# Masks, exponentials and reciprocals of an attention pair, spread over three successive steps of an attention and MoE kernel

## Chip, cores and metric

One core of a Trainium2 chip. The time is the device time of one execution, in microseconds; a lower time is better. The profile is one execution, with its own time.

## What is computed

```python
# windowed attention: 4 batches, 8 heads, 576 positions, head_dim 64
scores = scale * q @ k.T                       # only 0 <= row - col < 64 is kept
attn = exp(scores - max) / (sum(exp) + 1e-9)
x = (attn @ v) as rows                         # 2304 x 512
# gated product without a nonlinearity
x = ((x @ w1) * (x @ w2)) @ w3 @ w_out         # 512 -> 1024 -> 1024 -> 512
# top-1 of 8 experts
e = argmax(x @ w_gate); s = softmax prob of e * sigmoid(x @ w_output_gate)[e]
out = s * (relu(x @ ew1[e]) @ ew2[e])          # 512 -> 1024 -> 512
```

## The kernel before

Every large product is made of three matmuls (`product3`): each float32 operand is split in a high part (h, made by ScalarE as a rounding copy) and a low part (l, what is left, made by the vector engine or, for four pieces of w2 and two of w1, by GpSimd). A tile that ScalarE, the vector engine and TensorE hand round therefore passes ScalarE (copy), vector engine (subtract), and then TensorE.

Attention works in **pairs**: two heads by two blocks side by side, 3 windows of 64 rows each, six pairs p = 0 to 5 to a batch. A pair passes these calls:

- `score(p)`, TensorE: 24 small matmuls into two banks
- `masks(p)`, vector engine, L1002: for each of two halves a scaled sum with the mask (sm, L1011) and a lay (prob, L1015), then the negated row maxima (nmx, L1017). `score(p + 1)` waits until both sm of p have left the banks.
- `exps(p)`, ScalarE, L814: six exponentials with their sums (L818)
- `weigh(p)`, vector engine, L1032: 1e-9 added to the sums (L1035), reciprocals (rec, L1037)
- `normal(p)`, GpSimd, L1440: prob times rec (L1443)
- `turn(p)`, TensorE, L581: three transposes of prob; `turn_out(p)`, vector engine, four products into pT (L1027)
- `value(p)`, TensorE, L590: 24 small matmuls; `value_hi(p)` (ScalarE, L823) and `value_lo(p)` (vector engine, L1041) split the result into x, transposed. `value(p + 1)` waits for `value_lo(p)`.

The attention of the first batch lies in the **fold stage** (29 to 98 us and a little ahead of it). There TensorE multiplies w3 with w_out in 16 half products (`w_order`, steps i), each of which ScalarE and the vector engine split into Wh and Wl; meanwhile w3, w1 and w2 are loaded and split too (`hi_w3`, `lo_w3`, `hi_w12`, `lo_w12`). The other three batches lie each in a **chunk** of 384 rows of x (there are six chunks; three carry no attention). A chunk has 14 steps e: eight hidden tiles (e = 0 to 7), then six row tiles. In hidden tile f TensorE makes the two products of x with w1 and w2; ScalarE copies the first (a_sb, L890), the vector engine multiplies the second with it (ab_f, L1140), ScalarE rounds (abh, L892), the vector engine subtracts (abl, L1142). A row tile (L655) runs over eight parts f of abh and abl with W; in the first one TensorE waits, part by part, for abl of tile f. Row tiles of the kind n = 1 come first (e = 8 to 10); their result is copied out by the vector engine, that of n = 0 by ScalarE.

Every engine runs its own list of calls, in order, and waits on semaphores. The order is written by hand, by functions from the step to the pair whose call stands behind (or ahead of) the step's own work:

| call | engine | pair in step e, before |
|---|---|---|
| score | TensorE | 0 ahead of step 0; e/2 + 1 at even e |
| masks | vector engine | 0 ahead of step 0; e/2 + 1 at even e |
| exps | ScalarE | 0 ahead of step 0; e/2 + 1 at even e |
| weigh | vector engine, ahead of the step's own work | 0 at e = 1; e/2 at even e from 2 |
| turn, turn_out | TensorE, vector engine | e/2 - 1 at even e from 2 |
| value, value_hi, value_lo | TensorE, ScalarE, vector engine | e/2 - 2 at even e from 4; the last in step 13 |

In the fold stage the same holds for e = i - 2, with a few steps written out (`fold_scored`, `fold_weighed`). GpSimd's `normal` follows `fold_weighed` there, and `lo_w12` stands behind it in the steps 3, 6, 8, 10, 11 and 12. In a chunk GpSimd has only the `normal` calls and the stores of x. SyncE issues the loads; they wait for scores and values that have left their buffers. Within a step the vector engine takes its own work, then turn_out, value_lo, masks; ScalarE its own work, value_hi, exps.

Of the kernel before, what the change touches and what calls it, by code (L numbers as in the profile page):

```python
# [29 lines left out]
def build(nc, B, H, S, qT_in, kT_in, v_in, w1, w2, w3T_in, w_out, w_outT, w_gates, ew1, ew2, out):  # L30
# [41 lines left out]
    with ctx:  # L72
# [192 lines left out]
        def scored(e):  # L265
            return e // 2 + 1 if e % 2 == 0 and e // 2 + 1 < NP else None
# [4 lines left out]
        def valued(e):  # L271
            return e // 2 - 2 if e % 2 == 0 and e >= 4 else None

        def weighed(e):
            return 0 if e == 1 else e // 2 if e >= 2 and e % 2 == 0 and e // 2 < NP else None

        LAST = NP - 1

# [29 lines left out]
        def row_bank(cc, i):  # L308
            return bank[(2 * cc + i) % 4]
# [7 lines left out]
        def fold_scored(i):  # L317
            return i - 2 if i in (2, 3) else scored(i - 2) if i > 3 else None

        def fold_weighed(i):  # L320
            return {3: 0, 5: 1}.get(i, i // 2 - 1 if i >= 6 and i % 2 == 0 and i // 2 - 1 < NP else None)


        w3_steps = {1: 3, 5: 4, 7: 5, 9: 6, 11: 7}
# [12 lines left out]
        def w_bank(i):  # L337
            return bank[i % 4]
# [470 lines left out]
        def _(act):  # L809
# [4 lines left out]
            def exps(b, p):  # L814
                act.wait_ge(nmx_ok, b * NP + p + 1)
                for i in range(6):
                    pr, c = prob[p % 2][:, i * WIN:(i + 1) * WIN], p % 2 * 6 + i
                    ex_i = act.activation(pr, pr, ACT.Exp, bias=nmx[:, c:c + 1], accum_out=sums[:, c:c + 1])  # L818
                ex_i.then_inc(exp_ok, 1)
# [34 lines left out]
            for i, (it, n) in enumerate(w_order):  # L854
                def own():
                    first, end = PARTS[n]
                    if i == 3:
                        act.wait_ge(g1_done, 1)
                        for j in range(0, KF, 2):
                            g = act.activation(woh_pair(j, DM, WXC), bank[4][:, j * LG:(j + 2) * LG].rearrange("p (j c) -> p j c", c=LG),  # L860
                                               ACT.Copy)
                        g.then_inc(g1_hi, 1)
                    act.wait_ge(W_done, w_count(it, n))
                    act.activation(Wh[:, it * WXC + first:it * WXC + end], w_bank(i)[:, 0:end - first],
                                   ACT.Copy).then_inc(W_hi, 1)

                if i == len(w_order) - 1:
                    value_hi(0, LAST, 0)
                own()
                if i >= 2 and valued(i - 2) is not None:  # L870
                    value_hi(0, valued(i - 2), 0)
                if i in w3_steps:
                    hi_w3(w3_steps[i])
                if i == 2:
                    hi_wo(1)
                if fold_scored(i) is not None:
                    exps(0, fold_scored(i))
                if i in w12_steps:
                    hi_w12(w12_steps.index(i))

# [6 lines left out]
            def chunk(cc, c, batches, b, parity, final):  # L887
                def hidden_tile(f):
                    act.wait_ge(a_done, cc * KF + (f + 1))
                    act.activation(a_sb[f % 2][:, :], hidden_bank(cc, f, 0)[:, 0:CH], ACT.Copy).then_inc(a_ok, 1)  # L890
                    act.wait_ge(ab_ok, cc * KF + (f + 1))
                    act.activation(abh[:, f * CH:(f + 1) * CH], ab_f[f % 2][:, :], ACT.Copy).then_inc(ab_hi, 1)  # L892

                def row_tile(i, n, tt):
                    if n == 0:
                        act.wait_ge(xA_done, cc * CT + (tt + 1))
                        act.wait_ge(x_free, cc + 1)
                        act.activation(x_sb[tt][:, 0:HALF], row_bank(cc, i)[:, 0:HALF], ACT.Copy).then_inc(xA_ok, 1)

                def attend(e):  # L900
                    if b is not None and valued(e) is not None:
                        value_hi(b, valued(e), parity)
                    if b is not None and scored(e) is not None:
                        exps(b, scored(e))

                if b is not None:
                    exps(b, 0)
                for f in range(KF):
                    hidden_tile(f)
                    attend(f)  # L910
                if final:
                    for part in range(2):
                        for p in range(NP1):
                            split_hi(0, part, p)
                            if (part, p) == (1, 1):
                                xs_out(0, bank[7])
                for n, tt, i in row_tiles:
                    if b is not None and KF + i == NSTEP - 1:
                        value_hi(b, LAST, parity)
                    row_tile(i, n, tt)  # L920
                    attend(KF + i)
# [76 lines left out]
        def _(dve):  # L998
# [79 lines left out]
            for i, (it, n) in enumerate(w_order):  # L1078
                if i == 3:
                    dve.wait_ge(const_ok, 2)  # L1080
                if i == 2:
                    dve.wait_ge(const_ok, 1)

                def own():
                    if i - 1 in w3_steps:
                        lo_w3(w3_steps[i - 1])
                    if i == 3:
                        lo_wo(1)
                    if fold_weighed(i) is not None:
                        weigh(0, fold_weighed(i))  # L1090
                    if i >= 1:
                        weight_splits(i - 1)
                    first, end = PARTS[n]
                    if i == 3:
                        dve.wait_ge(g1_hi, 1)
                        for j in range(0, KF, 2):
                            g = wo_lo_out(j, DM, WXC, bank[4][:, j * LG:(j + 2) * LG].rearrange("p (j c) -> p j c", c=LG))
                        g.then_inc(g1_lo, 1)
                    dve.wait_ge(W_hi, w_count(it, n))
                    ws = slice(it * WXC + first, it * WXC + end)  # L1100
                    dve.tensor_tensor(Wl[:, ws], w_bank(i)[:, 0:end - first], f32(Wh[:, ws]), ALU.subtract).then_inc(W_lo, 1)

                if i == len(w_order) - 1:
                    value_lo(0, LAST, 0)
                own()
                if i >= 2 and turned(i - 2) is not None:
                    turn_out(0, turned(i - 2), 0)
                    turn_out(0, turned(i - 2), 1)
                if i >= 2 and valued(i - 2) is not None:
                    value_lo(0, valued(i - 2), 0)  # L1110
                if fold_scored(i) is not None:
                    masks(0, fold_scored(i))
            weight_splits(len(w_order) - 1)


# [5 lines left out]
            def chunk(cc, c, batches, b, parity, final):  # L1121
# [4 lines left out]
                def attend(e):  # L1126
                    if b is not None and turned(e) is not None:
                        turn_out(b, turned(e), 0)
                        turn_out(b, turned(e), 1)
                    if b is not None and valued(e) is not None:  # L1130
                        value_lo(b, valued(e), parity)
                    if b is not None and scored(e) is not None:
                        masks(b, scored(e))

                def hidden_tile(f):
                    weights(f)
                    fc = slice(f * CH, (f + 1) * CH)
                    dve.wait_ge(b_done, cc * KF + (f + 1))
                    dve.wait_ge(a_ok, cc * KF + (f + 1))
                    dve.tensor_tensor(ab_f[f % 2][:, :], hidden_bank(cc, f, 1)[:, 0:CH], a_sb[f % 2][:, :], ALU.mult).then_inc(ab_ok, 1)  # L1140
                    dve.wait_ge(ab_hi, cc * KF + (f + 1))
                    dve.tensor_tensor(abl[:, fc], ab_f[f % 2][:, :], f32(abh[:, fc]), ALU.subtract).then_inc(ab_lo, 1)  # L1142

                def row_tile(i, n, tt):
                    weights(KF + i)
                    if n == 1:
                        dve.wait_ge(xB_done, cc * CT + (tt + 1))
                        dve.wait_ge(x_free, cc + 1)
                        dve.tensor_copy(x_sb[tt][:, HALF:DM], row_bank(cc, i)[:, 0:HALF])
                        dve.tensor_copy(L[:, bass.ds(cc * (CT * LG) + tt * LG, LG)], row_bank(cc, i)[:, HALF:HALF + LG]).then_inc(xB_ok, 1)  # L1150

                if b is not None:
                    masks(b, 0)
# [415 lines left out]
```

## Time and profile before

| | us |
|---|---|
| median of 3 runs (lowest, highest) | 752.13 (749.43, 752.37) |
| the profiled execution | 752.49 |
| its span, first to last instruction | 750.7 |
| TensorE busy | 711.7 |
| vector engine / ScalarE / GpSimd busy | 372.8 / 266.7 / 120.1 |

The mean granted TensorE clock of the span is 0.979 of full speed. The table shows how much each engine has to do, not who waits for whom; a time in the rows counts from the span's start. The fold stage ends near 98 us, the three chunks with attention run from 98 to about 171, from 222 to about 295 and from 295 to about 368, the last chunk ends near 475, and the expert stage takes the rest.

### The profile page before, as it was taken

To read this page: it belongs to the slowest core of one execution; us is meant where nothing else is said; L and a number is where in the kernel's file an instruction comes from. 1 tells how busy PE (TensorE), PEld (TensorE's weight loads), DVE (VectorE), ACT (ScalarE), POOL (GpSimd) and SP (SyncE) were. 2 spreads that over 40 slices of the span, in tenths; PEclk is the share of its full clock that TensorE was granted. 3 is DMA by queue.
4 is the path that set the end of the run, shared out by engine and by line. 5 is a ranking of instruction groups with operands and counts; after the bars stand their busy time and mean duration, and the time that the engine had idled before them with its cause. 6 is when DMAs were issued, how large, how long until landed. Compare 5 with 4: busy or idle time off the path is not lost.

```text
span 750.7 us, 15001 instructions
## 1 busy us (share of the span) xinstructions
PE 711.7 (95%) x5075; PEld 647.8 (86%) x5076; DVE 372.8 (50%) x711; ACT 266.7 (36%) x651; POOL 120.1 (16%) x179
## 2 busy tenths in 40 slices
PE   8987699799999979997999999999999999999997
PEld 6986599689999968996999999878888888888886
DVE  4567756552215664576221257865355654562211
ACT  4442533322203422333121125535255544462212
POOL 7112400010000000000000000222122222221211
PEclk9999999899999989999999999999999999999999
DMA  9765112041012123210510104374447572711110
GB/s 339 246 228 166 35 44 58 22 147 37 1 43 64 37 83 100 64 37 22 194 73 1 43 4 165 127 269 154 154 141 237 186 241 83 233 34 43 31 54 29
DMA packets 44590, 80.12 MB, mean 107 GB/s; under 512 B 4413, under 2 KB 24893, under 8 KB 44544
## 3 DMA queue, kind: packets, MB, share of 16 engines
q1 hardware_dynamic: 39504, 64.01, 26.1%
q0 software_dynamic: 5040, 15.47, 5.9%
q8 instruction: 32, 0.52, 0.3%
q14 instruction: 14, 0.11, 0.0%
HBM read 70.03 MB, written 10.49 MB: 107 GB/s over the span
## 4 chain that ended last, share of the span: by engine, by line
PE 69%; DVE 18%; ACT 9%; issue 2%; DMA 1%; POOLq 0%; DVEq 0%; SPq 0%; ACTq 0%
PE bank L484 20%; PE bank L486 20%; PE bank L485 19%; ACT prob L818 6%; DVE pT L1027 5%; DVE sm L1011 3%; PE bank L759 3%; DVE prob L1015 2%; DVE ab_f L1140 2%; ACT abh L892 2%; DVE nmx L1017 2%; PE bank L600 1%; PE bank L737 1%; DVE abl L1142 1%; DVE xTl L1041 1%
## 5 line engine op out<-in xcount | busy, mean ns | idle before, releaser
L484 PE MATMUL bank<-Wh,abh 128*128 128x272 f32 (+1 forms) x288 | 84.7, 294 | 14.8 <-DVE abl L1142 14.8
L818 ACT ACTIVATE prob<-prob,nmx 128x64 f32<-128x64 f32 x144 | 48.2, 335 | 109.9 <-DVE nmx L1017 109.9
L486 PE MATMUL bank<-Wh,abl 128*128 128x272 f32 (+1 forms) x288 | 82.6, 287 | 0.0
L485 PE MATMUL bank<-Wl,abh 128*128 128x272 f32 (+1 forms) x288 | 82.5, 287 | 0.0
L1118 DVE TENSOR_TENSOR wbuf<-raw,wbuf 128x1024 f32 (+1 forms) x64 | 75.3, 1220 | 12.5 <-ACT wbuf L884 12.4
L1140 DVE TENSOR_TENSOR ab_f<-bank,a_sb 128x384 f32<-128x384 f32 x48 | 26.5, 552 | 105.3 <-PE bank L486 66.5
L1319 DVE TENSOR_TENSOR hTl<-bank,hTh 128x512 fp32r<-128x512 f32 x44 | 28.4, 685 | 97.7 <-ACT hTh L934 97.7
L484 PE MATMUL bank<-wbuf,hTh 128*128 (+1 forms) x176 | 70.7, 402 | 0.4 <-issue 0.4
L484 PE MATMUL bank<-wbuf,xsTh 128*128 (+1 forms) x176 | 70.4, 400 | 0.1
L484 PEld LDWEIGHTS bank<-Wh,abh 128*128 128x128 f32 x288 | 54.8, 190 | 16.9 <-DVE abl L1142 15.5
L486 PE MATMUL bank<-wbuf,hTl 128*128 (+1 forms) x176 | 68.8, 391 | 0.0
L486 PE MATMUL bank<-wbuf,xsTl 128*128 (+1 forms) x176 | 68.6, 390 | 0.0
L485 PE MATMUL bank<-wbuf,xsTh 128*128 (+1 forms) x176 | 68.6, 390 | 0.0
L485 PE MATMUL bank<-wbuf,hTh 128*128 (+1 forms) x176 | 68.4, 389 | 0.0
L484 PE MATMUL bank<-xTh,w1h 128*128 128x384 f32 x192 | 66.0, 344 | 0.0
L485 PE MATMUL bank<-xTl,w1h 128*128 128x384 f32 x192 | 64.3, 335 | 0.0
L486 PE MATMUL bank<-xTh,w1l 128*128 128x384 f32 x192 | 64.2, 334 | 0.0
L486 PE MATMUL bank<-xTh,w2l 128*128 128x384 f32 x192 | 64.2, 334 | 0.0
L484 PE MATMUL bank<-xTh,w2h 128*128 128x384 f32 x192 | 64.1, 334 | 0.0
L485 PE MATMUL bank<-xTl,w2h 128*128 128x384 f32 x192 | 64.1, 334 | 0.0
L884 ACT ACTIVATE wbuf<-raw 128x1024 f32 (+1 forms) x64 | 63.9, 1054 | 0.0
L1027 DVE TENSOR_TENSOR pT<-bank,side 64x384 f32<-64x384 f32 x96 | 53.1, 554 | 14.1 <-PE bank L587 12.3
(218 smaller groups left out, 1468.8 us busy)
## 6 DMA issues: line engine op xcount, KB each, us to landing
raw<-in_expert_w SPq DMA_DIRECT2D x64, 512.0 KB, 4.4
qT<-in_qT SPq DMA_DIRECT2D x24, 192.0 KB, 3.0
kT<-in_kT SPq DMA_DIRECT2D x24, 192.0 KB, 3.8
x_rows<-x_sb POOLq DMA_DIRECT2D x18, 256.0 KB, 2.3
w3r<-in_w3T SPq DMA_DIRECT2D x8, 512.0 KB, 5.2
wo<-in_w_out SPq DMA_DIRECT2D x8, 256.0 KB, 8.1
woT<-in_w_outT SPq DMA_DIRECT2D x4, 512.0 KB, 9.1
vA<-in_v SPq DMA_DIRECT2D x16, 128.0 KB, 2.1
```

The costliest lines, as they stand in the source:

```text
L484: pe.matmul(dst, lh, rh, start=first, stop=False)
L485: pe.matmul(dst, lh, rl, start=False, stop=False)
L486: return pe.matmul(dst, ll, rh, start=False, stop=last)
L759: mm = pe.transpose(bank[3 + n][:, (f % 4) * P:(f % 4 + 1) * P], h_sb[:, f * P:(f + 1) * P], ident[:, :])
L818: ex_i = act.activation(pr, pr, ACT.Exp, bias=nmx[:, c:c + 1], accum_out=sums[:, c:c + 1])
L884: act.activation(wbuf[:, bass.ds(wcol(e, part, 0, c * PC), PC)], raw[part * NP1 + c][:, :], ACT.Copy).then_inc(ew_hi[part], 1)
L892: act.activation(abh[:, f * CH:(f + 1) * CH], ab_f[f % 2][:, :], ACT.Copy).then_inc(ab_hi, 1)
L1011: dve.scalar_tensor_tensor(sm[:, :], score_bank(h)[:, 0:3 * P], SEQ_SCALE, mask[:, 0:3 * P] if unit_of(p)[1] == 0 else mask[:, P:4 * P], A ...
L1027: cut = dve.tensor_tensor(pT[buf_of(p, h)][w * WIN:(w + 1) * WIN, :].rearrange("p (i r c) -> p i r c", r=2, c=WIN), bank[4][rows, 0:3 * P] ...
L1118: dve.tensor_tensor(wbuf[:, bass.ds(wcol(e, part, 1, c * PC), PC)], raw[part * NP1 + c][:, :], f32(wbuf[:, bass.ds(wcol(e, part, 0, c * PC ...
L1140: dve.tensor_tensor(ab_f[f % 2][:, :], hidden_bank(cc, f, 1)[:, 0:CH], a_sb[f % 2][:, :], ALU.mult).then_inc(ab_ok, 1)
L1319: dve.tensor_tensor(hTl[last][:, cols], bank[3 + n][:, :], f32(hTh[last][:, cols]), ALU.subtract).then_inc(hT_lo, 1)
```

## The change

The masks of pairs 1 to 5 stand in the odd step behind the even one that ends with their scores (`laid`), the exponentials in the even step behind that (`raised`, for pair 0 behind step 0's own work and no longer ahead of it), the reciprocals in the odd step behind that (`weighed`), and they come behind the step's own work on the vector engine, no longer ahead of it. Pair 0's masks stay where they were. In the fold stage the same functions hold for i - 2, with the first steps written out; there GpSimd's `normal` takes the new steps too, so that it comes behind `lo_w12` of an earlier step more often: the order of the last three becomes lo_w12(4), lo_w12(5), normal(5). Scores, turns and values keep their steps, and so do all of TensorE's and SyncE's calls.

```diff
+        def laid(e):
+            return (e + 1) // 2 if e % 2 and (e + 1) // 2 < NP else None
+
+        def raised(e):
+            return e // 2 if e % 2 == 0 and e // 2 < NP else None
+
         def weighed(e):
-            return 0 if e == 1 else e // 2 if e >= 2 and e % 2 == 0 and e // 2 < NP else None
+            return e // 2 if e % 2 and e // 2 < NP else None
...
+        def fold_laid(i):
+            return i - 2 if i in (2, 3) else laid(i - 2) if i > 3 else None
+
+        def fold_raised(i):
+            return 0 if i == 2 else raised(i - 2) if i > 3 else None
+
         def fold_weighed(i):
-            return {3: 0, 5: 1}.get(i, i // 2 - 1 if i >= 6 and i % 2 == 0 and i // 2 - 1 < NP else None)
+            return weighed(i - 2) if i > 2 else None
...
-                if fold_scored(i) is not None:
-                    exps(0, fold_scored(i))
+                if fold_raised(i) is not None:
+                    exps(0, fold_raised(i))
...
-                    if b is not None and scored(e) is not None:
-                        exps(b, scored(e))
-
-                if b is not None:
-                    exps(b, 0)
+                    if b is not None and raised(e) is not None:
+                        exps(b, raised(e))
...
-                    if fold_weighed(i) is not None:
-                        weigh(0, fold_weighed(i))
                     if i >= 1:
                         weight_splits(i - 1)
...
                     dve.tensor_tensor(Wl[:, ws], w_bank(i)[:, 0:end - first], f32(Wh[:, ws]), ALU.subtract).then_inc(W_lo, 1)
+                    if fold_weighed(i) is not None:
+                        weigh(0, fold_weighed(i))
...
-                if fold_scored(i) is not None:
-                    masks(0, fold_scored(i))
+                if fold_laid(i) is not None:
+                    masks(0, fold_laid(i))
...
-                    if b is not None and scored(e) is not None:
-                        masks(b, scored(e))
+                    if b is not None and laid(e) is not None:
+                        masks(b, laid(e))
...
                 def hidden_tile(f):
-                    weights(f)
...
                     dve.tensor_tensor(abl[:, fc], ab_f[f % 2][:, :], f32(abh[:, fc]), ALU.subtract).then_inc(ab_lo, 1)
+                    weights(f)
...
                 def row_tile(i, n, tt):
-                    weights(KF + i)
                     if n == 1:
...
+                    weights(KF + i)
```

## Rows read from the trace of the kernel before

**Rows 1.** The page's first part: busy us, share and instructions of each engine

```profile
PE 711.7 (95%) x5075; PEld 647.8 (86%) x5076; DVE 372.8 (50%) x711; ACT 266.7 (36%) x651; POOL 120.1 (16%) x179
```

**Rows 2.** TensorE's waits: releaser, us in total, times, longest us

```profile
PE bank L484 <- DVE abl L1142: 14.8, 3, 4.9
PE bank L484 <- DVE w3l L1048: 7.8, 3, 3.5
PE bank L600 <- DVE xTl L1041: 5.2, 4, 2.3
```

**Rows 3.** Timeline of TensorE, first and third attention chunk: start, us, instruction

```profile
128.14 0.33 PE L484 MATMUL bank<-xTh,w1h 128*128 128x384 f32 x1
...
132.30 0.49 PE L587 MATMUL bank<-ident,prob 128*128 128x128 f32 x3
...
134.38 0.44 PE L484 MATMUL bank<-xTh,w1h 128*128 128x384 f32 x1
...
138.65 0.28 PE L484 MATMUL bank<-Wh,abh 128*128 128x272 f32 x1
...
141.16 0.29 PE L486 MATMUL bank<-Wh,abl 128*128 128x272 f32 x1
146.38 0.59 PE L484 MATMUL bank<-Wh,abh 128*128 128x272 f32 x1 [4.92 <-DVE abl L1142]
...
150.96 0.59 PE L484 MATMUL bank<-Wh,abh 128*128 128x272 f32 x1
...
338.35 0.29 PE L486 MATMUL bank<-Wh,abl 128*128 128x272 f32 x1
...
347.58 0.39 PE L484 MATMUL bank<-Wh,abh 128*128 128x272 f32 x1
```

**Rows 4.** Busy us by window: PE, PEld, DVE, ACT, POOL; granted clock; DMA

```profile
29.00:98.00 69.00, 55.50 (x570) 51.27 (x566) 46.00 (x87) 27.86 (x91) 19.29 (x11) 0.90 0.45 142
98.00:140.00 42.00, 42.00 (x376) 40.16 (x369) 26.33 (x58) 15.54 (x65) 3.32 (x4) 1.00 0.16 45
...
146.00:154.00 8.00, 7.62 (x73) 6.85 (x74) 6.26 (x15) 0.80 (x3) 0.83 (x1) 0.60 0.23 64
```

**Rows 5.** Timeline of the vector engine, steps 6 and 7 of the same chunk

```profile
136.65 2.27 DVE L1027 TENSOR_TENSOR pT<-bank,side 64x384 f32<-64x384 f32 x4
...
139.43 0.55 DVE L1011 SCALAR_TENSOR_TENSOR sm<-bank,mask 128x384 f32<-128x384 f32 x1
...
141.46 0.55 DVE L1017 TENSOR_REDUCE nmx<-prob 128x6 f32<-128x384 f32 x1
144.62 0.56 DVE L1140 TENSOR_TENSOR ab_f<-bank,a_sb 128x384 f32<-128x384 f32 x1 [2.60 <-ACT a_sb L890]
145.76 0.56 DVE L1142 TENSOR_TENSOR abl<-ab_f,abh 128x384 fp32r<-128x384 f32 x1 [0.59 <-ACT abh L892]
```

**Rows 6.** Timeline of ScalarE, the same steps

```profile
142.04 0.35 ACT L818 ACTIVATE prob<-prob,nmx 128x64 f32<-128x64 f32 x1 [5.53 <-DVE nmx L1017]
...
144.05 0.47 ACT L890 ACTIVATE a_sb<-bank 128x384 f32<-128x384 f32 x1
```

**Rows 7.** Timeline of the vector engine, fold stage

```profile
67.26 0.44 DVE L1101 TENSOR_TENSOR Wl<-bank,Wh 128x272 fp32r<-128x272 f32 x1 [3.39 <-ACT Wh L864]
...
82.84 2.35 DVE L1035 TENSOR_SCALAR sums<-sums 128x6 f32<-128x6 f32 x1
...
88.76 1.21 DVE L1055 TENSOR_TENSOR w1l<-w1r,w1h 128x1024 fp32r<-128x1024 f32 x1
```

**Rows 8.** Timeline of GpSimd: fold stage, and first attention chunk

```profile
81.80 3.37 POOL L1453 TENSOR_TENSOR w1l<-w1r,w1h 128x1024 fp32r<-128x1024 f32 x1
...
135.21 0.83 POOL L1443 TENSOR_TENSOR prob<-prob,rec 128x384 f32<-128x384 f32 x1 [10.66 <-DVE rec L1037]
```

**Rows 9.** Single lines: count, ns min/median/max, first and last start (us)

```profile
L1015 DVE TENSOR_TENSOR prob<-sm x48: 357/358/361, 22.5 to 349.7; 128x192 f32<-128x192 f32 x48
...
L1048 DVE TENSOR_TENSOR w3l<-w3r,w3h x3: 2178/2179/2223, 55.8 to 80.7; 128x1024 fp32r<-128x1024 f32 x3
```

## The prediction

> **What bounds the kernel now.** The page first: TensorE is busy 711.7 us of a span of 750.7, the vector engine half of it, ScalarE 36% [rows 1]. So TensorE sets the time, and what a change of order can give is its idle 39 us and what it runs slowly. The list of TensorE's waits says whom it waited for [rows 2]: 14.8 us in three waits for abl, the low part of a hidden tile (vector engine); 7.8 us in three for w3l; 5.2 us in four for xTl; the rest is smaller. The three waits for abl are one in each of the three chunks that carry attention, the others but for some of xTl's lie in the fold stage.
>
> TensorE's timeline of the first such chunk shows the place [rows 3]. Hidden tile 7 ends at 138.65, the first row tile runs its parts 0 to 6 and then stands until 146.38, 4.92 us, for part 7. What follows is also slow: turn, values and scores take 2.08 us in step 6 (132.30 to 134.38), but with three matmuls ahead of them 4.58 us here (146.38 to 150.96), where 2.5 would do; over 146 to 154 the granted clock is 0.60, against 1.00 over the 42 us before [rows 4]: the lower level, 1.2 GHz, held for a while behind the idle stretch.
>
> Why abl of tile 7 comes so late is read from the vector engine's and ScalarE's timelines [rows 5, 6]. In step 6 the vector engine does turn_out(2), value_lo(1) and then masks(4), up to 142.0. ScalarE takes exps(4) directly behind them, until 144.1, and only then copies a_sb of tile 7, though that tile had left TensorE at 138.65. The product starts at 144.62 and abl at 145.76, each as soon as the one before it is there. Scores, masks, exponentials and the next tile's copy stand in one line through three engines, about 6 us too long.
>
> The fold stage, 29 to 98 us, has 13.5 us of idle TensorE and a granted clock of 0.90 [rows 4]. The pattern is the same: the split Wl waits 3.39 us for ScalarE's Wh [rows 7], which by the order of calls is queued behind the exponentials of the masks just ended and a weight copy, and the w3l split that TensorE wants is queued behind Wl.
>
> **The change, part by part.** No instruction is added or removed; three calls change their step on the vector engine and ScalarE, and GpSimd's fold order follows. SyncE's and TensorE's orders stand. So the sum is made of starts and ends.
>
> *Masks one step later, exponentials two steps behind the scores.* I follow steps 5 to 8 of the first attention chunk, with each duration as the rows have it. Step 5's tile ends at 128.1 [rows 3]. Product 0.55, ScalarE's abh 0.53 and abl 0.56, with hand-overs of about 0.05, end at 129.9; exps(2) were done before, so the reciprocals are out at 130.3 and masks(3) (two sm of 0.56, two lays of 0.36, one maximum of 0.55 [rows 5, 9], 2.55 in all with hand-overs) fill 130.3 to 132.9. Step 6's tile ends at 132.3; its product starts at 132.9 rather than 135.05, abl ends at 134.6, turn_out(2) and value_lo(1) (2.27 and 0.56) at 137.5, and nothing more is queued. ScalarE does value_hi(1) and exps(3), 2.1 us, by 136.5, then a_sb of tile 7 when its first half is out, near 136.6. Tile 7 ends at 138.65, its product starts at 138.75 and abl ends at 140.45. TensorE asks for it at 141.3. The 4.92 us are gone, and with them the low clock.
>
> The price of one chunk, from 141.3 to where TensorE is again at full clock, which in the first chunk is six matmuls into the second row tile, at 152.44 (1.5 us after 150.96 [rows 3]): 11.1 us before. After: 0.4 for the last three matmuls, 2.1 for turn, values and scores as in step 6, 0.1 for the new wait below, 0.8 for six matmuls: 3.4. Gain 7.7 us. The second chunk has the same rows. In the third the row tile behind the scores is at full clock from 347.58 [rows 3], 9.1 us after the last matmul that ran before the wait was through, at 338.5; after, 2.6; gain 6.5. Three chunks: **21.9 us**.
>
> What is late next? masks(4) now stand in step 7, 140.9 to 143.7; TensorE's score(5) needs only their two sm, by 142.6, and starts near 143.1. The first row tile's copy, turn_out(3) and value_lo(2) follow until 147.0; value(3) asks near 150.5. No stall. The wait for xTl in the last row tile (part of the 5.2 us [rows 2]) hangs on turn(5), turn_out(5) and value_lo(4), whose order is unchanged: it stays.
>
> *Reciprocals behind the step's own work.* They move behind product and abl, some 1.6 us after the tile's end. GpSimd's normalising takes 0.83 us [rows 8]. In a hidden step: tile end, +1.75 for abl, +0.4 reciprocals, +0.1, +0.83 is 3.1 us, and the next step's TensorE work is 4.2 us: 1.1 us to spare before the turn. In step 8 the row tile takes 3.05 us: the turn asks at 141.7, prob is ready at 141.8. So 0.1 us, once a chunk. The other row steps wait for no abl and have more room. Queued behind the reciprocals are that step's masks, of which the schedule has the slack above.
>
> *Both engines at once.* The fold stage shows them excluding each other [rows 7 to 9]: the w3l split at 80.7 took 2.18 us, though w1l of the same size takes 1.21; it ended 1.1 us behind the moment at which GpSimd passed to its next instruction, 81.80, and that one then took 3.37; and the sums instruction, usually 0.16, took 2.35, until GpSimd was done. No lay ran slow before: 357 to 361 ns in all 48 [rows 9]. After, GpSimd's normalising starts just when masks start, so a lay can wait; bounds per pair are 0 and about 0.3 us (0.83 less the 0.56 of sm ahead of it). I take 0.3; it lies in the slack. In the Trainium skill, "SBUF — State Buffer", section "Who interferes with whom", the shared port pair is an exclusive lock, and a vector instruction with two SBUF inputs contends with a GpSimd one that reads SBUF, while tensor_reduce does not. The trace's w3l row agrees; by this rule the lays do wait, and without it the sum would be the same, since the 0.3 us is covered. This is the rule that speaks against the change where GpSimd's instructions are 2.4 us long, in the fold.
>
> *The fold stage.* Worked in the same way, from 29 us. ScalarE's Wh no longer stands behind exponentials whose masks just ended, so the periods of 12.5 us (three w3l splits from 55.8 to 80.7 [rows 9]) fall towards TensorE's own, about 8.4: 3.05 and 2.9 for two halves, 2.2 for turn, values and scores. The w3l splits are done before TensorE asks, but for the last, 0.5. The new waits are at the turns: reciprocals for pairs 2 to 5 are now queued behind Wl, when ScalarE has just finished a weight's high part and GpSimd is in its 2.4 us low part. They wait for it. For pair 2: TensorE's step i = 6 ends near 40.0 (no 2.0 us wait now), value(0) and score(3) near 42.2, i = 7 and 8 near 48.2, where turn(2) asks; ScalarE has exps(2) from 41.8 to 43.9 and the weight's high part to 44.9; GpSimd's low part holds until 47.3, the reciprocals end at 47.7, normal at 48.6. The same for the next pairs gives turns 2, 3, 4 late by 0.5, 0.6 and 0.6 us, turn(5) by some 3.9 (here GpSimd's order has changed too: its last w1l piece goes ahead of pair 5), and value(5) by 1.0. Left: 7.0 us idle. Before: 13.5 idle and up to 0.10 of 69 us, 6.9, lost to the low clock [rows 4]. An idle stretch of 3.9 us keeps perhaps half of the clock loss, 3. Gain 13.5 + 6.9 - 7.0 - 3 = 10.4, taken as **10 us**. Bounds: 0 if each turn waits a whole GpSimd instruction and the clock stays low, 14 if the last turn comes with the others.
>
> Whether each weight lands in time for the faster fold these rows don't say; TensorE's list has no wait for a transfer near their size [rows 2], and a late one would be part of rival 1. Chunks without attention and the expert stage only start sooner.
>
> Sum: 21.9 + 10 is 32 us off the profiled run's 752.49 (span 750.7 and 1.8 around it), which is 0.4 above the median 752.13. Off the median: **720 us**.
>
> **The rivals.**
> 1. *The fold gives nothing.* The wait moves from w3l to GpSimd's prob. For it: the 2.35 us sums row, and the order, which puts a GpSimd piece beside most reciprocals. Against: GpSimd is busy 19.3 of 69 us there [rows 4]. Fold gain 0 to 4: 726 to 730.
> 2. *The stall moves in the chunks also.* The reciprocals come some 1 us later than worked, and four turns a chunk stand about 1 us each, perhaps with the low clock: 12 us back. 732 to 745. Against: turns 0 to 2 have 1.1 us to spare.
> 3. *Slower.* One mechanism: the turn waits for late reciprocals at every one of 24 pairs. It decides from 32/24 = 1.3 us idle at each, that is reciprocals 2.4 us later than worked; at 1.6 us: 759. The fold's lock can do this, the chunks' 0.83 us instruction can't.
> 4. *No effect.* Tile 7's abl is held by something that the move leaves, or score(5) then stands for masks(4) as long: 750 to 754. Against: the rows give a gap-free chain from masks(4) to abl.
>
> **How the numbers follow.** Forecast (713 to 726) 0.62; rival 1 0.20; rival 2 0.10; rival 4 0.04; rival 3 0.04. The range 713 to 734 takes the forecast, rival 1 and the foot of rival 2; below it one would need nearly all that both stages lose, 21.9 and 20.4 us, which is 710. What a measurement can tell from none is 0.5%, 3.8 us. Faster: the forecast and rivals 1 and 2, 0.92. Same 0.04, slower 0.04.
>
> **What would show it.** In the profile after: the waits for abl L1142 gone or under 0.5 us in all; ScalarE's long waits for the maxima short; granted clock 1.00 through each attention chunk; a chunk some 7 us shorter; in the fold the w3l waits at most 1 us, and a new group, TensorE's transposes waiting for GpSimd's prob, of 3 to 7 us. The prediction is wrong if that group holds over 12 us, if abl's wait is still there, or if score waits for sm.

## The result, and the profile after

The changed kernel takes 718.63 us (median of 4 runs, 715.89 to 718.94) against 750.88 (4 runs, 749.43 to 752.37) for the kernel before: ratio 0.9562, 95% interval 0.9528 to 0.9596, 4.4% faster. 720 was predicted. The profiled execution took 718.94 us with a span of 717.2.

The page's first part and its chain of work, against [rows 1]: TensorE is busy 701.5 us, 10 less than before (matmuls that no longer run at the low clock), and its share of the span is 98%.

```profile
PE 701.5 (98%) x5075; PEld 639.1 (89%) x5076; DVE 378.0 (53%) x711; ACT 268.5 (37%) x651; POOL 119.9 (17%) x179
...
PE 91%; DVE 4%; DMA 1%; issue 1%; ACT 1%; POOL 1%; POOLq 0%; DVEq 0%; ACTq 0%
```

TensorE's waits after, against [rows 2] (releaser, us in total, times, longest). The rows for abl and for w3l are gone. The group that the prediction named, transposes behind GpSimd's prob, has grown to four waits; before it held one, of 2.0 us at 42.13:

```profile
PE bank L599 <- POOL prob L1453: 4.6, 4, 3.4
PE bank L612 <- DVE xTl L1051: 2.8, 3, 0.9
PE bank L574 <- DVE prob L1081: 1.5, 1, 1.5
```

ScalarE's waits for the maxima, 109.9 us in 24 before, are 3.1 us in three. No wait of the scores for sm is listed.

TensorE's timeline at the place of the 4.92 us wait of [rows 3]. Row tile 0 starts at 125.08 and runs its 24 matmuls on end; the turn follows at 128.35:

```profile
125.08 0.28 PE L496 MATMUL bank<-Wh,abh 128*128 128x272 f32 x1
...
127.73 0.29 PE L496 MATMUL bank<-Wh,abh 128*128 128x272 f32 x1
127.85 0.29 PE L497 MATMUL bank<-Wl,abh 128*128 128x272 f32 x1
127.98 0.29 PE L498 MATMUL bank<-Wh,abl 128*128 128x272 f32 x1
128.35 0.52 PE L599 MATMUL bank<-ident,prob 128*128 128x128 f32 x3
```

The vector engine there, against [rows 5]: step 6 ends with xTl at 123.39, the product of tile 7 waits for TensorE and no longer for ScalarE, abl starts 1.36 us after TensorE turned to the row tile (7.1 us before), and reciprocals and masks follow it:

```profile
123.39 0.56 DVE L1051 TENSOR_TENSOR xTl<-bank,xTh 128x384 fp32r<-128x384 f32 x1
125.28 0.56 DVE L1149 TENSOR_TENSOR ab_f<-bank,a_sb 128x384 f32<-128x384 f32 x1 [1.34 <-PE bank L498]
126.44 0.56 DVE L1151 TENSOR_TENSOR abl<-ab_f,abh 128x384 fp32r<-128x384 f32 x1 [0.59 <-ACT abh L904]
126.91 0.16 DVE L1045 TENSOR_SCALAR sums<-sums 128x6 f32<-128x6 f32 x1
127.11 0.19 DVE L1047 RECIPROCAL rec<-sums 128x6 f32<-128x6 f32 x1
127.22 0.53 DVE L1021 SCALAR_TENSOR_TENSOR sm<-bank,mask 128x384 f32<-128x384 f32 x1
127.78 0.64 DVE L1025 TENSOR_TENSOR prob<-sm 128x192 f32<-128x192 f32 x1
```

Busy time and granted clock by window, against [rows 4]. The fold stage has the low clock in part, the chunk not at all:

```profile
28.00:84.00 56.00, 51.15 (x566) 47.55 (x558) 48.47 (x89) 29.04 (x90) 20.35 (x12) 0.94 0.54 172
84.00:126.00 42.00, 42.00 (x379) 40.08 (x378) 27.19 (x57) 16.73 (x67) 2.49 (x3) 1.00 0.18 51
126.00:134.00 8.00, 7.91 (x97) 7.32 (x97) 6.69 (x16) 2.88 (x14) 0.83 (x1) 1.00 0.30 84
```

A chunk with attention opens with its score of pair 0. These rows of TensorE's timeline after (the second and third from other windows) give the stages:

```profile
84.08 0.89 PE L587 MATMUL bank<-kT,qT 64*64 64x128 f32 x24
...
200.89 0.89 PE L587 MATMUL bank<-kT,qT 64*64 64x128 f32 x24
...
266.83 0.89 PE L587 MATMUL bank<-kT,qT 64*64 64x128 f32 x24
```

Before, the same three scores start at 97.57, 221.97 and 294.82. So:

| stretch (us) | before | after | gain | predicted |
|---|---|---|---|---|
| to the first chunk (loads and fold) | 97.57 | 84.08 | 13.5 | 10 |
| first chunk with attention and the one behind it | 124.40 | 116.81 | 7.6 | 7.7 |
| second | 72.85 | 65.94 | 6.9 | 7.7 |
| third, to the next chunk's first product (367.02 and 332.69) | 72.20 | 65.86 | 6.3 | 6.5 |
| all that follows, where the orders are the same | 383.7 | 384.5 | -0.8 | 0 |

The second term was read too high. The prediction took its rows to be those of the first chunk. The wait is as long, but the low clock (1.2 GHz) began sooner. By windows of 0.25 us it runs from 145.5 to 152.4 in the first chunk, from 268.3 to 275.2 in the second and from 343.5 to 346.9 in the third. Of the second one 2.4 us had passed while TensorE still stood, of the first 0.9. TensorE's timeline before, second chunk:

```profile
270.70 0.59 PE L484 MATMUL bank<-Wh,abh 128*128 128x272 f32 x1 [4.94 <-DVE abl L1142]
...
275.29 0.39 PE L484 MATMUL bank<-Wh,abh 128*128 128x272 f32 x1
```

At half speed TensorE loses half of the low time behind the wait. The wait plus that half, less 0.25 us for the later turn(3), gives 7.7, 6.9 and 6.3 us, against the 7.6, 6.9 and 6.3 measured.

### The profile page after: what moved, and what is told of

Same layout as the page of the kernel before. It is cut to its first block, busy times and chain, and to the rows that moved or that the text cites. A ratio compares the mean times of both kernels' runs of the same rounds, so it can differ in the third digit from the quotient of the medians.

```text
span 717.2 us, 15001 instructions
## 1 busy us (share of the span) xinstructions
PE 701.5 (98%) x5075; PEld 639.1 (89%) x5076; DVE 378.0 (53%) x711; ACT 268.5 (37%) x651; POOL 119.9 (17%) x179
## 4 chain that ended last, share of the span: by engine, by line
PE 91%; DVE 4%; DMA 1%; issue 1%; ACT 1%; POOL 1%; POOLq 0%; DVEq 0%; ACTq 0%
PE bank L496 27%; PE bank L498 26%; PE bank L497 26%; PE bank L771 3%; PE bank L587 3%; PE bank L612 2%; DVE pT L1037 2%; PE bank L749 1%; PE bank L599 1%; DMA xs<-x_rows,gidc 1%; DVE prob L1025 1%; PE bank L509 1%; PE bank L731 1%; DMA w3r<-in_w3T 1%; DVE w3l L1058 1%
## 5 line engine op out<-in xcount | busy, mean ns | idle before, releaser
L904 ACT ACTIVATE abh<-ab_f 128x384 fp32r<-128x384 f32 x48 | 25.2, 525 | 111.8 <-DVE ab_f L1149 111.8
L896 ACT ACTIVATE wbuf<-raw 128x1024 f32 (+1 forms) x64 | 63.9, 1054 | 0.0
```

The source lines that it names most:

```text
L896: act.activation(wbuf[:, bass.ds(wcol(e, part, 0, c * PC), PC)], raw[part * NP1 + c][:, :], ACT.Copy).then_inc(ew_hi[part], 1)
```

## The experiments

The ratios are against runs of the kernel before on the same chip. The median of the kernel before differs by up to 2 us from chip to chip, so kernels measured on different chips are compared by ratio.

### One stage at a time

`chunks_only` gives the fold stage its order of before:

```diff
         def fold_laid(i):
-            return i - 2 if i in (2, 3) else laid(i - 2) if i > 3 else None
+            return fold_scored(i)
...
         def fold_raised(i):
-            return 0 if i == 2 else raised(i - 2) if i > 3 else None
+            return fold_scored(i)
...
         def fold_weighed(i):
-            return weighed(i - 2) if i > 2 else None
+            return {3: 0, 5: 1}.get(i, i // 2 - 1 if i >= 6 and i % 2 == 0 and i // 2 - 1 < NP else None)
...
+                    if fold_weighed(i) is not None:
+                        weigh(0, fold_weighed(i))
                     if i >= 1:
                         weight_splits(i - 1)
...
-                    if fold_weighed(i) is not None:
-                        weigh(0, fold_weighed(i))
```

> The change in the three chunks with attention alone; the fold stage keeps the order of before. By the forecast's theory the gain is the sum of two stages that don't touch each other, and this is the chunks' part: 21.9 us by the prediction, so about 729 us, with no wait of TensorE for abl L1151 and the three w3l waits (7.8 us) still there. The rival, that the two stages share one gain (a stall removed in the fold only shifts the chunks' start), would give a sum of both parts well away from 32 us.

Measured: 729.95 us, ratio 0.9730 (0.9703 to 0.9757), 20.3 us off. No wait for abl; w3l's are there:

```profile
PE bank L496 <- DVE w3l L1058: 8.6, 3, 3.5
```

`fold_only` does the reverse (in the chunks `scored`, the old `weighed`, and the reciprocals ahead of the step's work).

> The change in the fold stage alone; the chunks keep the order of before. The stage ended at 97.6 us before and at 84.1 us after, 13.4 us earlier, against 10 predicted. By the additive theory this kernel takes 737 to 739 us, has three waits for abl of 4.9 us each, and no w3l wait. If chunks and fold share a gain: under 8 us, above 743.

Measured: 738.22 us, ratio 0.9835 (0.9810 to 0.9860), 12.1 off the 750.30 of those runs. TensorE waits for abl as before:

```profile
PE bank L499 <- DVE abl L1158: 14.8, 3, 4.9
PE bank L602 <- POOL prob L1459: 4.6, 4, 3.4
```

20.3 and 12.1 make 32.4; the whole change gave 32.3. The stages add.

### One move undone

`exps_behind_masks`: the exponentials directly behind their masks, one step later than before.

```diff
         def fold_raised(i):
-            return 0 if i == 2 else raised(i - 2) if i > 3 else None
+            return fold_laid(i)
...
-                    if b is not None and raised(e) is not None:
-                        exps(b, raised(e))
+                    if b is not None and laid(e) is not None:
+                        exps(b, laid(e))
+
+                if b is not None:
+                    exps(b, 0)
```

> The masks one step later as in the change, but each pair's exponentials directly behind them in the same step (the exponentials' move undone). Theory L, the line through three engines must be cut in both places: masks, exponentials, the next a_sb and product stand in one line again, about 12 us for two steps against 10.5 of TensorE, so the chunks fall back by 5 to 7 us each and the fold by some 4: 735 to 745, with TensorE waiting for prob at the turns and for abl again. Theory M, it is enough that the masks are out of step 6: 719, no wait for abl.

Measured: 736.58 us, ratio 0.9802 (0.9765 to 0.9840): theory L. More than half of the gain goes. By the scores of pair 0, which start at 20.05, 86.13, 208.45 and 280.02, the first two chunk stretches are 5.5 and 5.6 us longer than in the changed kernel, as expected, and the fold is 2.2 us longer (66.1 against 63.9 from the first score on), where some 4 was expected. TensorE's waits in this kernel:

```profile
PE bank L599 <- POOL prob L1456: 14.6, 14, 4.3
PE bank L496 <- DVE abl L1154: 3.9, 3, 1.3
```

The delay grows from pair to pair, as worked out: in the first chunk the turns wait 0.59, then 1.04, then tile 7's abl is late by 1.29:

```profile
111.02 0.52 PE L599 MATMUL bank<-ident,prob 128*128 128x128 f32 x3 [0.59 <-POOL prob L1456]
122.80 0.52 PE L599 MATMUL bank<-ident,prob 128*128 128x128 f32 x3 [1.04 <-POOL prob L1456]
133.28 0.39 PE L496 MATMUL bank<-Wh,abh 128*128 128x272 f32 x1 [1.29 <-DVE abl L1154]
```

`masks_in_scores_step`: masks as before the change (`scored`, `fold_scored`), exponentials and reciprocals as in it.

```diff
         def fold_laid(i):
-            return i - 2 if i in (2, 3) else laid(i - 2) if i > 3 else None
+            return fold_scored(i)
...
-                    if b is not None and laid(e) is not None:
-                        masks(b, laid(e))
+                    if b is not None and scored(e) is not None:
+                        masks(b, scored(e))
```

> The masks in the step of their scores as before, the exponentials two steps behind the scores and the reciprocals as in the change (the masks' move undone). Theory E, ScalarE's copy behind the exponentials was the whole delay: the product of tile 7 waits only for masks(4), which end near 140 on the first chunk's old clock instead of 144.6, abl ends near 141.8, TensorE asks at 141.3: 0.3 to 1 us a chunk, 720 to 722 in all. Theory L, both moves are needed: waits for abl of 2 us and more a chunk with the low clock, 728 or more.

Measured: 725.28 us, ratio 0.9661 (0.9636 to 0.9686). Neither theory as it stood, and the time lies between their ranges: in the chunks E holds. No wait for abl is left, and the scores of pair 0 start at 90.67, 208.07 and 274.61, so the first two stretches take 117.40 and 66.54 us, 0.6 more than in the changed kernel. But the fold ends 6.6 us later (90.67 against 84.08); 0.8 of that lies ahead of its first score (20.98 against 20.20), so 5.8 is the order's. There the masks now meet GpSimd's weight part. The vector engine's timeline, and GpSimd's:

```profile
46.23 0.56 DVE L1021 SCALAR_TENSOR_TENSOR sm<-bank,mask 128x384 f32<-128x384 f32 x1
46.83 2.57 DVE L1025 TENSOR_TENSOR prob<-sm 128x192 f32<-128x192 f32 x1
...
50.55 1.20 DVE L1058 TENSOR_TENSOR w3l<-w3r,w3h 128x1024 fp32r<-128x1024 f32 x1
```

```profile
46.77 2.42 POOL L1463 TENSOR_TENSOR w2l<-w2r,w2h 128x1024 fp32r<-128x1024 f32 x1 [5.07 <-ACT w2h L847]
50.71 1.72 POOL L1453 TENSOR_TENSOR prob<-prob,rec 128x384 f32<-128x384 f32 x1 [1.53 <-DVE rec L1047]
```

The lay issued just behind GpSimd's low part takes 2.57 us where 0.36 is usual; the normalising issued just behind the w3l split takes 1.72 where 0.83 is usual. TensorE stands 2.47 us at that turn, with the low clock behind it.

### The reciprocals' place, and how much room they have

`weigh_ahead`: the reciprocals in the change's steps, but ahead of the step's own work, in the fold and in the chunks (shown for the hidden tiles; row tiles and fold are changed in the same way).

```diff
                 def hidden_tile(f):
+                    weights(f)
                     fc = slice(f * CH, (f + 1) * CH)
...
                     dve.tensor_tensor(abl[:, fc], ab_f[f % 2][:, :], f32(abh[:, fc]), ALU.subtract).then_inc(ab_lo, 1)
-                    weights(f)
```

> As the changed kernel, but the reciprocals ahead of the step's own work on the vector engine, in their new (odd) steps. If their place behind that work costs anything, this is faster: the prediction's 0.1 us a chunk at turn(3). In the fold stage they would come 0.8 us sooner, but GpSimd's low part, which starts one ScalarE instruction behind the exponentials, holds them there as well. Expected: 718 to 719, the changed kernel's time. Against: if the vector engine now waits for exponentials ahead of each product, over 722.

Measured: 715.73 us, ratio 0.9518 (0.9502 to 0.9534). Expected to be the same, it was some 3 us faster (the two ratios' intervals just overlap; the spans are 713.7 and 717.2). The three chunks are 0.3 us shorter each (116.51 and 65.63 for the first two stretches); the fold ends at 82.48, 1.6 sooner. I had overlooked what stands behind the reciprocals of pair 5: in the changed kernel it is the vector engine's own low part of w1, which then keeps GpSimd's normalising waiting. With the reciprocals ahead of it, a Wl split stands between them, and normal takes its 0.83 us. How much of the 1.6 us is due to that is taken up below. The last 1.0 us of the difference lie behind the third chunk, where the two kernels run in the same order; it isn't ascribed.

`late_reciprocals` makes prob late on purpose, by one more GpSimd instruction ahead of each normalising in the chunks:

```diff
             def normalise(b):
                 for p in range(NP):
+                    pool.wait_ge(rec_ok, b * NP + p + 1)
+                    pw = prob[p % 2][:, :].rearrange("p (g c) -> p g c", c=P)
+                    then(pool.tensor_tensor(pw, pw, ones[:, :].unsqueeze(1).broadcast_to([P, 3, P]), ALU.mult))
                     normal(b, p)
```

> As the changed kernel, but in the chunks GpSimd multiplies prob by ones (0.83 us more, same values) ahead of each of the 18 normalisings. A measure of the room that the prediction worked out: 1.1 us before the turn in a hidden step, about none in step 8. Theory: in each chunk turn(3) waits some 0.8 to 1.2 us and the other turns hardly, and the vector engine's lays wait longer, hidden: 721 to 723. If there is no room anywhere (the rival that every turn waits), 18 turns at 0.8 us and more: 733 and above. If there is room in step 8 too: 718.6.

Measured: 722.92 us, ratio 0.9624 (0.9603 to 0.9646), 4.7 us slower by the ratios; the first two stretches are 118.76 and 67.88, 1.9 longer each. The added instruction takes 1.01 us and puts the normalising off by 1.1, not by 0.83. GpSimd's timeline:

```profile
127.12 1.01 POOL L1459 TENSOR_TENSOR prob<-prob,ones 128x384 f32<-128x384 f32 x1 [8.82 <-DVE rec L1047]
128.22 0.83 POOL L1453 TENSOR_TENSOR prob<-prob,rec 128x384 f32<-128x384 f32 x1
```

TensorE's timeline, turn(0) and turn(3):

```profile
97.80 0.52 PE L599 MATMUL bank<-ident,prob 128*128 128x128 f32 x3
...
129.19 0.52 PE L599 MATMUL bank<-ident,prob 128*128 128x128 f32 x3 [1.18 <-POOL prob L1453]
```

Turn(3) is the only turn of the chunk for which the profile lists a wait, but not the only one that is late. Counted from the chunk's first score, turns 0, 1 and 2 start at 14.67, 24.57 and 35.32 us against 14.47, 24.14 and 34.65 in the changed kernel: each hidden step with a turn has become 0.2 us longer, and each of these turns starts some 0.15 us after its normalising ends (97.65 to 97.80 at turn(0)). So the room in a hidden step is about 0.9 us, and 1.1 goes past it by 0.2. These three delays are 0.7 us; with the 1.1 at turn(3) they are nearly all of the 1.9.

### The wait that is left, at turn(5) of the fold

The changed kernel's longest wait, on TensorE and then on the vector engine and GpSimd:

```profile
75.89 0.87 PE L599 MATMUL bank<-ident,prob 128*128 128x128 f32 x3 [3.42 <-POOL prob L1453]
```

```profile
65.82 1.76 DVE L1025 TENSOR_TENSOR prob<-sm 128x192 f32<-128x192 f32 x1
...
72.68 1.05 DVE L1045 TENSOR_SCALAR sums<-sums 128x6 f32<-128x6 f32 x1
73.77 0.19 DVE L1047 RECIPROCAL rec<-sums 128x6 f32<-128x6 f32 x1
73.87 1.19 DVE L1065 TENSOR_TENSOR w1l<-w1r,w1h 128x1024 fp32r<-128x1024 f32 x1
```

```profile
71.33 2.37 POOL L1463 TENSOR_TENSOR w1l<-w1r,w1h 128x1024 fp32r<-128x1024 f32 x1 [3.97 <-ACT w1h L847]
74.03 1.71 POOL L1453 TENSOR_TENSOR prob<-prob,rec 128x384 f32<-128x384 f32 x1 [0.33 <-DVE rec L1047]
```

The sums wait for GpSimd's w1 part; then the normalising waits for the vector engine's. Three kernels act on these waits.

`normal5_first`:

```diff
-                if fold_weighed(i) is not None:
+                if fold_weighed(i) is not None and i != 13:
                     normal(0, fold_weighed(i))
+                if i == 12:
+                    normal(0, LAST)
```

> As the changed kernel, but GpSimd takes pair 5's normalising in the fold stage ahead of its last w1 low part. The changed kernel's longest wait is there: TensorE idle 3.42 us at turn(5), and its clock at the lower level until 82. By the theory that GpSimd's order and the exclusion of the two engines make this wait, the sums instruction takes 0.16 instead of 1.05 us and normal is done near 74 to 75.1 instead of 75.7: idle 1.5 to 2.6 us, and less of the low clock: 713 to 717. The rival, that pair 5's exponentials are what is late: no change, 718.6.

Measured: 716.04 us, ratio 0.9526 (0.9510 to 0.9541). The sums at turn(5) take 0.16 again, and TensorE's wait is 2.49.

`normal5_first_w1l_behind`, which also puts `weight_splits` behind Wl:

```diff
-                    if i >= 1:
-                        weight_splits(i - 1)
...
                     dve.tensor_tensor(Wl[:, ws], w_bank(i)[:, 0:end - first], f32(Wh[:, ws]), ALU.subtract).then_inc(W_lo, 1)
+                    if i >= 1:
+                        weight_splits(i - 1)
                     if fold_weighed(i) is not None:
```

> As the run before, and the vector engine's w1 low part, which stands directly behind pair 5's reciprocals and excludes GpSimd's normalising for 1.2 us, comes behind the next Wl. By the exclusion theory normal is then done near 74.0, the idle stretch at turn(5) is 1.5 us or less and the clock stays up: 712 to 715, and faster than the run before by up to 2 us. If that low part didn't hold GpSimd: the same time as the run before.

Measured: 715.05 us, ratio 0.9511 (0.9495 to 0.9526). GpSimd's normalising takes 0.83 (1.71 in the run before), now the vector engine's w1 part is the one that waits, and TensorE's wait is 1.61. The interval of the ratio overlaps that of the run before: the shorter wait is shown by the trace, a shorter time isn't.

```profile
73.02 0.83 POOL L1453 TENSOR_TENSOR prob<-prob,rec 128x384 f32<-128x384 f32 x1 [5.77 <-DVE rec L1047]
```

```profile
73.18 1.75 DVE L1065 TENSOR_TENSOR w1l<-w1r,w1h 128x1024 fp32r<-128x1024 f32 x1
```

`pool_quarters` leaves the order and cuts GpSimd's weight parts:

```diff
-                ws = slice(kt * FF, (kt + 1) * FF)
                 pool.wait_ge(w12_hi, i + 1)
-                pool.tensor_tensor(wl[:, ws], wr[:, ws], f32(wh[:, ws]), ALU.subtract).then_inc(w12_lo, 1)
+                for part in range(4):
+                    ws = slice(kt * FF + part * FF // 4, kt * FF + (part + 1) * FF // 4)
+                    lo = pool.tensor_tensor(wl[:, ws], wr[:, ws], f32(wh[:, ws]), ALU.subtract)
+                lo.then_inc(w12_lo, 1)
```

> As the changed kernel, but each of GpSimd's six low parts of 1024 columns is made by four instructions of 256 columns. If the two engines exclude each other instruction by instruction, the vector engine comes in between two of them: the five sums instructions of 1.05 to 1.14 us fall under 0.7, the lay of 1.76 too, and the three waits of 0.4 us at turns 2, 3 and 4 go or halve; turn(5) keeps most of its wait, as GpSimd's own order stays: 717 to 718.5. The rival, that sums waits for GpSimd's results or shares bandwidth with it: 1.1 us as before and no change.

Measured: 716.18 us, ratio 0.9523 (0.9507 to 0.9539), just under the expected range. The longest sums instruction falls from 1144 to 527 ns and the longest lay from 1766 to 891, as they should if the vector engine gets in between two of GpSimd's instructions; that the sums wait for GpSimd's whole result is ruled out (the line's count, ns min/median/max, starts):

```profile
L1045 DVE TENSOR_SCALAR sums<-sums x24: 159/165/527, 28.6 to 321.2; 128x6 f32<-128x6 f32 x24
```

The waits at turns 2, 3 and 4, which were expected to go or halve, grew from 0.4 to 0.6 us, since GpSimd needs 2.83 us for the four parts instead of 2.40 and normalises behind them. That at turn(5) fell from 3.42 to 2.21:

```profile
75.06 0.52 PE L599 MATMUL bank<-ident,prob 128*128 128x128 f32 x3 [2.21 <-POOL prob L1453]
```

`ahead_and_first` joins `weigh_ahead` and `normal5_first`; `ahead_first_quarters` adds the quarters.

> The changed kernel with the reciprocals ahead of the step's own work, and GpSimd's normalising of pair 5 ahead of its last w1 low part. Each alone took some 3 us off. Both act on the same wait at turn(5), so they don't add: normal near 74.0, idle 1.6 us as with the w1 low part moved, 715. If their gains were of different waits: 712 to 713.

> The run before, and GpSimd's low parts in quarters. By the exclusion theory the lay of 1.75 us and the sums of 1.4 and 2.4 us get shorter, so the vector engine, on which the fold's end hangs, is 1 to 2 us earlier at pair 5: 713 to 714. If the four instructions' own cost (3.8 us instead of 2.4 for one part beside vector work) is what counts: no gain or up to 1 us slower.

Measured: 714.33 us, ratio 0.9507 (0.9486 to 0.9528), and 712.83, ratio 0.9488 (0.9467 to 0.9509). The first is no clear step beyond its two parts, as expected of gains at one wait: 1.31 us of it is left. The second is the fastest kernel of the study, 5.1% under the kernel before and, by intervals that don't meet, faster than the changed kernel; its interval does meet that of the first, so what the quarters add isn't clear of the noise. Turn(5) has no wait in it, but turns 2 to 4 have 0.6 us each. TensorE's waits for prob:

```profile
PE bank L599 <- POOL prob L1453: 1.8, 3, 0.6
```

How much of the 3 us that several of these kernels gained is their order's? The fold can be timed from its first score to the chunk's first score. It takes 63.9 us in the changed kernel, but 62.8 in both `fold_only` and `late_reciprocals`, which have the same orders in the fold and nearly the same wait at turn(5); the difference is how long the low clock lasted (last section). Against these two the fold gains 0.6 us in `weigh_ahead`, 0.7 in `pool_quarters`, 1.4 in `normal5_first`, 2.0 in `normal5_first_w1l_behind`, 1.8 in `ahead_and_first` and 3.2 in `ahead_first_quarters`. These are single traces.

## Why the prediction was right

**The stall and its cause** were right: masks(4), exps(4) and a_sb of tile 7 in one line. What the prediction did not ask is whether both moves are needed. In the chunks it is enough to move the exponentials (with the reciprocals), to 0.6 us a chunk (`masks_in_scores_step`); with masks and exponentials both one step later and still in one line, most of the gain is lost (`exps_behind_masks`). In the fold, against the changed kernel, leaving the masks where they were costs 5.8 us, and leaving the exponentials directly behind the masks 2.2. What the masks' move does there, by the rows of `masks_in_scores_step`, is to keep them away from GpSimd's weight parts.

**The total** is closer than its terms: 720 against 718.63. The chunks gave 1.6 us less than predicted (21.9 against 20.3 in `chunks_only`) and the fold 2.1 more (10 against 12.1 in `fold_only`). That the errors cancel is luck.

**The chunks' price.** The terms were 7.7, 7.7 and 6.5; measured are 7.6, 6.9 and 6.3. The second is the one that was read wrong, as shown with the table: its low clock ended 4.5 us behind the wait, not 6. The 0.1 us at turn(3) was too small: the turn starts 3.27 us after the row tile, where 3.05 was its own time. Prob is ready at 3.13 (the normalising that starts at 127.38 takes 0.83), and the 0.14 us from there to the turn was left out. Moving the reciprocals ahead brings 0.3 a chunk.

**The room behind the reciprocals** was put at 1.1 us in a hidden step and none in step 8. By `late_reciprocals` it is about 0.9 in a hidden step; the term left out is again the 0.15 us from normalising to turn. That step 8 has none was right.

**The lays wait for GpSimd's normalising**: 0.64 us instead of 0.36 for the first lay of a pair, 0.28 against the 0.3 taken, hidden as said. By the rule of the Trainium skill ("SBUF — State Buffer", section "Who interferes with whom") they had to; the trace agrees.

**The fold** was mis-sized: 10 us predicted, 12.1 by `fold_only`, 13.5 in the two profiles. Of the 13.5, 0.8 lies ahead of the change: score(0) starts at 20.20 instead of 21.00, and the other traces have one or the other too, whatever their order (20.0 to 20.4, or 21.0 to 21.1). The waits were placed right: turns 2, 3, 4 late by about 0.4 each (0.5, 0.6, 0.6 predicted), turn(5) by 3.42 (3.9). TensorE's idle time in 28 to 84 is 56.0 - 51.15 = 4.9 us, where 7.0 was the estimate: 1.0 less at the turns, 1.0 for the last value, whose wait for xTl didn't come, and 0.5 for the last w3l split, which came in time; 0.25 ahead of the first half product was not counted. The wait for xTl is missing in the traces with the low clock between turn(5) and the last value; in `weigh_ahead` and `normal5_first`, at full clock, it is 1.51 and 0.87. So the term at fault is the idle time left, 2 us too much.

The fold's clock term is uncertain: 0.06 of 56, 3.4, in the changed kernel's trace (3 predicted), but 0.03 of 56, 1.7, in that of `fold_only`. The prediction's sum, 13.5 + 6.9 - 4.9 less the clock term, gives 12.1 with the one and 13.8 with the other, so that 12.1 is also what `fold_only` measured proves little. The period of 8.4 us that the prediction named is not the sum of its parts either (3.05 + 2.9 + 2.2 = 8.15); the turns come 8.63 apart, 0.4 of it the new wait.

**The rivals.** 1 (fold gives nothing) fell with `fold_only`. 2 (the stall moves in the chunks) showed only as the 0.3 us. 3's mechanism exists: `exps_behind_masks` has 14 waits for prob, and still is 2% faster than before. 4 fell with the first profile.

## What to carry to other kernels

A call that hands from engine to engine should stand at each of them behind the work that others need sooner, one step of the main loop later each time, as long as its last user leaves room: here the hidden steps had 0.9 us to spare, and the shorter step 8 none. Look at what an in-order engine must finish ahead of the next tile's copy before counting its busy share: ScalarE was busy 36% and held up TensorE by 4.9 us. Where the vector engine and GpSimd work side by side on SBUF, look at which instruction of the one starts just behind a long one of the other. Cutting GpSimd's long instructions shortened the vector engine's waits here, but made GpSimd later; a gain in time from it alone isn't shown.

## What the runs showed of the hardware

The exclusion of vector engine and GpSimd goes by whole instructions and either side waits: a lay of 0.36 us took 2.57, a normalising of 0.83 took 1.72, and a sums instruction of 0.16 between 1.05 and 2.40, by how long the other still ran. Cutting GpSimd's instruction in four bounded the sums' wait at 0.53, though each quarter took 0.73 us by itself, four of them more than the 2.4 of the whole. The engine that began first isn't slowed: the GpSimd part beside the lay of 2.57 us took 2.42, against 2.40 elsewhere. In that way this differs from sharing a bandwidth.

TensorE's clock fell to the lower level (1.2 GHz) around or behind some waits and not behind others, and the length of the wait doesn't sort them. At turn(5) of the fold, by windows of 0.5 us:

| kernel | TensorE's wait (us) | low clock, from to |
|---|---|---|
| changed kernel | 3.42 | 75.2 to 82.0 |
| `fold_only` | 3.43 | 77.3 to 80.7 |
| `late_reciprocals` | 3.39 | 76.2 to 79.7 |
| `pool_quarters` | 2.21 | 76.1 to 79.5 |
| `weigh_ahead` | 2.54 | none |
| `normal5_first` | 2.49 | none |
| `normal5_first_w1l_behind` | 1.61 | none |

In the changed kernel it lasted 6.8 us, in the next three about 3.5, though the first three have the same orders there. So part of what a kernel seems to gain over the changed kernel is this difference: behind the wait the low clock cost the changed kernel's trace 3.1 us, half of the time from 75.9 to 82.0, and the next three some 1.7.
